# Folding x along the sequence, with the sequence factored as 32 x 94 instead of 64 x 47

## The chip, the cores and the metric

One Trainium2 chip, one of its NeuronCores. The metric is the device time of one launch in microseconds (us). TensorE is PE in the profile, its weight loads PEld; VectorE is DVE, ScalarE ACT, GpSimd POOL, and SyncE SP, which here only issues DMAs.

## The reference

`x` has the shape (2, 3008, 256). The first layer takes the real part of a two-dimensional discrete Fourier transform over the sequence (3008) and the features (256). Its 6016 rows pass a gated layer: rows are scaled to unit mean square (`rms`, with `rms_g`), `silu(xn @ w_gate) * (xn @ w_val) @ w_out` with an inner width of 1536, and then a second layer `h = x @ w_in; (h * cos(h)) @ w_out` with an inner width of 2048. All of it is float32.

```python
X = np.fft.fft(np.fft.fft(x, axis=1), axis=2).real
rms = np.sqrt(np.mean(x * x, axis=-1, keepdims=True) + 1e-06)
silu(xn @ w_gate) * (xn @ w_val) @ w_out      # xn = x / rms * rms_g
g = h * np.cos(h); g @ w_out                  # h = x @ w_in
```

## The kernel before

The transform of a real input is symmetric, so only the rows s and -s are computed as pairs: u is the part that the two share, v the part in which they differ, and the two tokens of a pair are u + v and u - v (`one_token`). The sequence is factored: position n1 * 47 + n2, frequency k1 + 64 * k2, with N1 = 64, N2 = 47; of the k1 only K1 = 33 are needed.

**First stage.** x stands in SBUF as (batch, n1) on 128 partitions. SP loads it in 11 chunks (`load_x`), VectorE folds the features of each chunk in place (L745, L748: x[d] and x[256-d] to their sum and difference), TensorE transforms over n1 (L386; for each of 47 n2 and both halves c of the features a matmul of 132 columns, behind `warm_up` passes), and ScalarE copies the result to `g_sb` (L541). TensorE then waits for `n1_out`, `feat_in` and `seq2_in`.

**Middle.** The loop over G takes two k1 at a time, 17 steps per batch. `features` (L402) transforms over the features (128 and 129 columns for each k1), `pq_copy` (VectorE, L767) takes its result from PSUM and adds the column of feature 128, and `sequence` (L416, L418) of the step before transforms over n2, with 47 and 94 columns. ScalarE copies u and v out (`uv_copy` L550, `row0_copy` L560), squares them for the mean (`square`, L572), and POOL adds the squares of u and v (`add_squares`, L957). `rms` (L430) sums over the features on TensorE, `mean_copy` (L580, L584) moves the means into rows of `stat`, one part at a time: 4 parts per batch, each with an issue of a DMA on ScalarE's queue. `add_epsilon` and `recip` (VectorE), `root` (ScalarE) and `inverse` (POOL) turn them into 1/rms, for three groups of rows.

In the same loop the weights are prepared, at steps that lists fix by hand (`WO1_AT`, `MIX_AT`, `WIN2_AT`). Every float32 weight is split in a rounded high part (ScalarE, L600, L606, L612) and the low rest (POOL, L933). For w1 VectorE first scales the two halves of the rows (L792, L793: `raw_a` by ga and by ga0) and then adds or subtracts the other half (L800, the mix). All 12 parts of w1 and all 6 of wo1 are ready before tile 0; of win2 4 of 8 are, and the others follow in tile 0.

SP's queue is in order: after `inv_done` 1 it stores 1/rms to DRAM (`store_inv`, L289), loads it back spread over the partitions (`load_inv`, L307), stores all of batch 0's u and v (`store_uv`, L298), waits for that (L303), and loads the first tile. POOL scales it (`scale_uv`, L976), ScalarE rounds it (`split_uv`, L616), POOL takes the rest (L1012) and increments `uv_split`, for which TensorE waits before `up1(0, 0)`.

**Tiles.** Six tiles of 502 pairs. In each, `up1` (12 steps of 4 x 3 passes, L442 to L444) computes gate and value, VectorE combines them (L832, L840, L841), ScalarE applies silu (L678), POOL multiplies (L1043), and high and low parts (L639, L817, L933) feed `down` two steps later; then `up2` and `down` do the same for the second layer, over 16 steps, with sin and squares for the cosine. Every product is of three matmuls (high by high, high by low, low by high). One mean, the last, is summed in tile 0, between the first halves of `up1(0, 1)`.

## Time and profile before

| what | value |
|---|---|
| median of 3 runs | 1018.89 us (1018.28 to 1018.94) |
| the profiled execution | 1018.42 us |
| its span, first to last instruction | 1016.7 us |
| busy: TensorE, VectorE, ScalarE, GpSimd | 1008.2, 759.1, 648.2, 368.6 us |
| granted TensorE clock | 1.000 |
| DMA traffic | 32.55 MB |

The times are from the profile; the 1.7 us between span and time lie outside the first and last instruction. A matmul of float32 is shown as two passes (x2). Busy times overlap where an instruction starts before the one in front of it has drained, so the distance of two starts says more than a duration.

### The profile page before, as it was taken

How to read it: one execution, taken by the hardware profiler on the slowest of the kernel's cores; microseconds unless marked ns; L12 is line 12 of the kernel's file. 1: busy time of each engine (PE TensorE's matmuls, PEld its weight loads, DVE VectorE, ACT ScalarE, POOL GpSimd, SP SyncE). 2: the span in 40 equal slices, each digit the busy share in tenths (PEclk: the TensorE clock that was granted, in tenths of full speed). 3: DMA queues.
4: the chain of work that ended last, by engine and by line, in shares of the span. 5: the costliest groups of instructions: out<-in, count | busy, mean ns of one | idle time of the engine just before them, and what ended most of it. 6: DMA issues, size and time to landing. Idle time of an engine off the chain costs nothing.

```text
span 1016.7 us, 13635 instructions
## 1 busy us (share of the span) xinstructions
PE 1008.2 (99%) x4780; PEld 841.4 (83%) x4780; DVE 759.1 (75%) x1059; ACT 648.2 (64%) x850; POOL 368.6 (36%) x302
## 2 busy tenths in 40 slices
PE   8999999999999999999999999999999999999998
PEld 8988788888888888888888888888888888888886
DVE  6785997776887776887676887676887676887665
ACT  6566567876446876446876447876447876447776
POOL 0486887102763002763002763002763002761000
PEclk9999999999999999999999999999999999999999
DMA  9611400000101000101000101000100000100001
GB/s 312 262 42 62 155 1 31 11 1 0 41 1 41 1 1 0 41 0 40 0 0 1 40 0 41 0 0 0 40 1 30 0 0 0 40 0 1 0 0 41
DMA packets 10277, 32.55 MB, mean 32 GB/s; under 512 B 2458, under 2 KB 6298, under 8 KB 9498
## 3 DMA queue, kind: packets, MB, share of 16 engines
q1 hardware_dynamic: 10102, 32.05, 9.0%
q8 instruction: 17, 0.28, 0.1%
q14 instruction: 26, 0.21, 0.1%
q10 hardware_dynamic: 132, 0.01, 0.0%
HBM read 22.78 MB, written 9.26 MB: 32 GB/s over the span
## 4 chain that ended last, share of the span: by engine, by line
PE 97%; DMA 1%; DVE 1%; ACT 0%; issue 0%; POOL 0%; SPq 0%; ACTq 0%; DVEq 0%
PE ps L442 30%; PE ps L443 30%; PE ps L444 30%; PE ps L402 3%; PE ps L418 2%; PE ps L386 2%; PE ps L416 1%; DMA x_sb<-x 1%; PE ps L430 1%; POOL work L1043 0%; SPq L262 0%; DVE pq L767 0%; ACT g_sb L541 0%; DVE dif_f L800 0%; ACT work L678 0%
## 5 line engine op out<-in xcount | busy, mean ns | idle before, releaser
L442 PE MATMUL ps<-h_hi,wo_hi 128*128 128x502 f32 x672 | 261.4, 389 | 0.5 <-DVE h_lo L817 0.5
L444 PE MATMUL ps<-h_hi,wo_lo 128*128 128x502 f32 x672 | 261.6, 389 | 0.0
L443 PE MATMUL ps<-h_lo,wo_hi 128*128 128x502 f32 x672 | 260.9, 388 | 0.0
L933 POOL TENSOR_TENSOR h_lo<-work,h_hi 128x502 fp32r<-128x502 f32 x92 | 101.7, 1114 | 381.0 <-ACT h_hi L654 381.0
L639 ACT ACTIVATE h_hi<-work 128x502 fp32r<-128x502 f32 x132 | 82.7, 626 | 189.3 <-POOL work L1043 189.3
L920 DVE SCALAR_TENSOR_TENSOR work<-work,ps 128x1004 f32<-128x1004 f32 (+1 forms) x109 | 117.2, 1075 | 97.6 <-ACT work L723 97.2
L906 DVE SCALAR_TENSOR_TENSOR work<-work,ps 128x1004 f32<-128x1004 f32 (+1 forms) x109 | 116.5, 1074 | 49.0 <-ACT work L709 49.0
L442 PE MATMUL ps<-x_hi,win_hi 128*128 128x502 f32 x384 | 150.0, 391 | 0.0
L443 PE MATMUL ps<-x_lo,win_hi 128*128 128x502 f32 x384 | 149.4, 389 | 0.0
L444 PE MATMUL ps<-x_hi,win_lo 128*128 128x502 f32 x384 | 149.1, 388 | 0.0
L442 PEld LDWEIGHTS ps<-h_hi,wo_hi 128*128 128x128 f32 x672 | 126.2, 188 | 27.2 <-issue 0.9
L444 PEld LDWEIGHTS ps<-h_hi,wo_lo 128*128 128x128 f32 x672 | 126.3, 188 | 25.8
L443 PEld LDWEIGHTS ps<-h_lo,wo_hi 128*128 128x128 f32 x672 | 126.2, 188 | 25.9
L832 DVE SCALAR_TENSOR_TENSOR plus<-u,w,ps 128x502 f32<-128x502 f32 x144 | 105.8, 734 | 52.1 <-PE ps L444 51.4
L709 ACT ACTIVATE work<-ps 128x1004 f32<-128x1004 f32 (+1 forms) x109 | 98.3, 907 | 60.5 <-PE ps L444 59.6
L718 ACT ACTIVATE work<-work 128x1004 f32<-128x1004 f32 (+1 forms) x109 | 102.7, 943 | 31.6 <-DVE work L906 30.8
L1043 POOL TENSOR_TENSOR work<-work,uv_t 128x502 f32<-128x502 f32 x72 | 99.1, 1397 | 49.5 <-DVE uv_t L841 44.5
L825 DVE TENSOR_TENSOR h_lo<-work,h_hi 128x502 fp32r<-128x502 f32 x172 | 111.1, 684 | 1.4
L654 ACT ACTIVATE h_hi<-work 128x1004 fp32r<-128x1004 f32 (+1 forms) x109 | 101.7, 939 | 14.3 <-PE ps L444 8.7
L723 ACT ACTIVATE work<-work 128x1004 f32<-128x1004 f32 (+1 forms) x109 | 102.8, 943 | 8.0
L1043 POOL TENSOR_TENSOR work<-work,work 128x502 f32<-128x502 f32 x60 | 84.4, 1427 | 36.3 <-DVE work L841 32.5
L442 PEld LDWEIGHTS ps<-x_hi,win_hi 128*128 128x128 f32 x384 | 72.2, 188 | 16.4 <-DVE work L920 1.6
(86 smaller groups left out, 1479.3 us busy)
## 6 DMA issues: line engine op xcount, KB each, us to landing
out<-y_sb SPq DMA_DIRECT2D x10, 502.0 KB, 3.0
x_sb<-x SPq DMA_DIRECT2D x6, 768.0 KB, 10.3
uv_t<-uv_dram SPq DMA_DIRECT2D x6, 502.0 KB, 3.6
uv_dram<-uv SPq DMA_DIRECT2D x2, 1457.0 KB, 8.9
win_raw<-win SPq DMA_DIRECT2D x1, 2048.0 KB, 14.8
wo_raw<-wo SPq DMA_DIRECT2D x1, 2048.0 KB, 9.7
raw_a<-w1a SPq DMA_DIRECT2D x1, 1536.0 KB, 21.9
wo_raw<-wo SPq DMA_DIRECT2D x1, 1536.0 KB, 24.5
```

What stands on the lines that cost most here:

```text
L442: nc.tensor.matmul(acc, w_hi, v_hi, start=start, stop=False)
L443: nc.tensor.matmul(acc, w_hi, v_lo, start=False, stop=False)
L444: return nc.tensor.matmul(acc, w_lo, v_hi, start=False, stop=stop)
L654: nc.scalar.activation(h_hi[j % 2][:, gs, 0:N], work[j % 4][:, gs, :], ACT.Copy).then_inc(hi_done, gs.stop - gs.start)
L718: nc.scalar.activation(work[j % 4][:, gs, :], work[j % 4][:, gs, :], ACT.Sin, scale=TURN / 2).then_inc(sin_done, gs.stop - gs.start)
L723: nc.scalar.activation(work[j % 4][:, gs, :], work[j % 4][:, gs, :], ACT.Square, scale=float(np.sqrt(2.0))).then_inc(sin2_done, gs.stop - ...
L825: nc.vector.tensor_tensor(h_lo[j % 2][:, g, 0:N], work[j % 4][:, g, :], h_hi[j % 2][:, g, 0:N].bitcast(F32), ALU.subtract).then_inc(hid_sp ...
L832: nc.vector.scalar_tensor_tensor(out=plus[m][:, :], in0=u128[:, :], scalar=w128[:, m * C1 + i:m * C1 + i + 1], in1=ps[:, bank_pair(m), 0:N ...
L906: nc.vector.scalar_tensor_tensor(out=buf, in0=buf, scalar=MAGIC, in1=pair, op0=ALU.subtract, op1=ALU.subtract).then_inc(frac_done, gs.stop ...
L920: nc.vector.scalar_tensor_tensor(out=buf, in0=buf, scalar=1.0, in1=pair, op0=ALU.subtract, op1=ALU.mult).then_inc(cos_done, gs.stop - gs.s ...
L933: nc.gpsimd.tensor_tensor(dst, src, hi.bitcast(F32), ALU.subtract).then_inc(s, 1)
L1043: nc.gpsimd.tensor_tensor(work[i % 3][:, g, :], work[i % 3][:, g, :], value[i % 2][:, g, :], ALU.mult).then_inc(h_done[g], 1)
```

## The change

x is folded along the sequence too. The host places x twice, as positions t and -t: on 128 partitions stand (position or its mirror, batch, n1), now with N1 = 32 and, of N2 = 94, the H = 48 first n2; VectorE adds to the features' fold a fold across the two feature orders, and the first transform takes 4 blocks (two folds, two batches) of 34 columns. K1 becomes 17. The tables carry the weight 1/2 where a position is its own mirror.

- First stage: 24 groups m of 512 columns instead of 47 of 256, in 10 chunks; per chunk three operations on VectorE instead of two; 48 matmuls of 136 columns instead of 94 of 132; two warm-up matmuls ahead of every chunk but the first.
- Middle: 34 steps of one k1. `features` keeps 128 and 129 columns, `sequence` has 94 and 188, and runs two steps behind; three PSUM banks for the first, four for the second, four slots of `pq`. ScalarE works on pairs of steps (17), with one split in two where the batches meet.
- Means: 9 parts (3 3 4 4 3 and 4 4 4 5 rows of k1), seven in the loop, two in tile 0.
- w1: `raw_b` is scaled once by gb0 (6 operations), then 12 mixes read `raw_a` and `raw_b` (the 6 others of the scaling are gone). Loads come in the order seq2 (first 8 k1), raw_b, seq2 (rest), wo1, raw_a.
- Half of w1's low parts (6), 2 of wo1's and all of win2 move from the middle into tile 0, on ScalarE and POOL.
- SP stores the first 6 rows of batch 0's u and v early, loads tile 0, stores the rest, and only then stores 1/rms and loads it.

The core of the diff:

```diff
-N1, N2 = 64, 47
+N1, N2 = 32, 94
+H = N2 // 2 + 1
...
-STEPS = (K1 + 1) // 2
-CHUNKS = [1, 2, 3, 3, 6, 6, 6, 6, 6, 6, 2]
+STEPS = K1
+CHUNKS = [1, 2, 3, 3, 3, 3, 3, 3, 2, 1]
+PARTS = [[3, 3, 4, 4, 3], [4, 4, 4, 5]]
...
+        RMS_AT = [8, 10, 14, 18, 22, 26, 30]
+        RMS_LATE = range(len(RMS_AT), MEANS)
...
-        MIX_AT = [6, 7, 9, 10, 12, 13, 15, 16, 18, 19, 21, 22]
-        WO1_AT = [3, 4, 5, 6, 9, 12]
-        WIN2_AT = 24
+        W1_ORDER = [0, 3, 1, 4, 2, 5]
+        SCALE_AT = [5, 6, 7, 8, 9, 10]
+        MIX_AT = [13, 14, 16, 17, 19, 20, 22, 23, 25, 26, 29, 31]
+        W1_HI_AT = [7, 9, 11, 13, 15, 16]
+        WO1_AT = [4, 5, 5, 6]
...
             load(feat[:, :], t_feat, feat_in)
-            load(seq2[0:SEQ_ROWS, :, :], t_seq2.rearrange("p (a k) -> p a k", a=K1), seq2_in)
+            load_seq2(slice(0, SEQ2_FIRST), seq2_in)
+            load(raw_b[:, :], w1b, raw_b_in)
+            load_seq2(slice(SEQ2_FIRST, K1), seq2_rest)
+            load(wo1_raw[:, :], wo1, wo1_in)
             load(raw_a[:, :], w1a, raw_a_in)
-            load(wo1_raw[:, :], wo1, wo1_in)
-            load(raw_b[:, :], w1b, raw_b_in)
...
+            store_uv(0, (slice(0, 1), slice(1, FIRST_ROWS)))
+            sp.wait_ge(uv_stored, UV_FIRST)
+            sp.wait_ge(pq_done, STEPS)
+            load_tile(0)
+            load_u128(0)
+            store_uv(0, (slice(FIRST_ROWS, K1 - 1), slice(K1 - 1, K1)))
             sp.wait_ge(inv_done, 1)
             store_inv(0, (slice(0, 1), slice(1, FIRST_ROWS)), 0)
             sp.wait_ge(inv_out, INV_OUT[0])
             load_inv(0)
-            store_uv(0)
-            sp.wait_ge(uv_stored, 48)
-            sp.wait_ge(pq_done, K1)
-            load_tile(0)
-            load_u128(0)
...
+                if G >= 4:
+                    pe.wait_ge(uv_row0, 2 * (G // 2 - 1))
+                if G == SEQ2_FIRST:
+                    pe.wait_ge(seq2_rest, 16)
+                bank = 4 + G % 4
...
+                if 0 < q < len(RMS_AT):
+                    pe.wait_ge(mean_out, q)
...
+            for G in range(LAST):
                 features(G)
+                if G >= 2:
+                    sequence(G - 2)
+                if G in RMS_AT:
+                    rms(RMS_AT.index(G))
+            sequence(LAST - 2)
...
             pe.wait_ge(uv_split, 1)
-            pe.wait_ge(w1_lo_done, 12)
-            pe.wait_ge(wo1_lo_done, 6)
...
+            for p in range(LAST // 2):
+                uv_copy(p)
+                row0_copy(p)
+                for q in parts_ending(p):
                     square(q)
+                for q in means_copied(p):
                     mean_copy(q)
+                split_step(p)
+                if p == 6:
                     root(0)
+                if p == 13:
                     root(1)
+                if p == 12:
                     split_uv(0)
...
                     if first and i == 0:
+                        for q in RMS_LATE:
+                            mean_copy(q)
+                    if first and i in (2, 3):
+                        wo1_part(WO1_EARLY + i - 2)
+                    if first and 4 <= i < 8:
+                        win2_part(2 * (i - 4))
+                        win2_part(2 * (i - 4) + 1)
...
+                nc.vector.tensor_tensor(part[:, :, 0:DIM], part[:, :, 0:DIM], part[:, :, DIM:XM], ALU.add
+                                        ).then_inc(even_done, 1)
+                dve.wait_ge(even_done, i + 1)
...
+            for G in range(LAST):
                 pq_copy(G)
                 split_step(G)
+                if G == 14:
                     add_epsilon(0)
+                if G == 16:
                     recip(0)
+                if G == 27:
                     add_epsilon(1)
+                if G == 30:
                     recip(1)
...
+                    if first and i < 6:
+                        w1_part(W1_EARLY + i)
+                    if first and 6 <= i < 8:
+                        wo1_part(WO1_EARLY + i - 6)
+                    if first and 8 <= i < 10:
+                        win2_part(i - 8)
```

`means_copied(p)` gives mean q to the pair p = (RMS_AT[q] - 2) / 2, and `parts_ending(p)` gives each part's square to the pair that holds its last row. On POOL the middle's order is now: `add_squares` 0, 1, wo1 0, squares 2, wo1 1 and 2, squares 3, wo1 3, `inverse(0)`, w1 0 and 1, squares 4, w1 2 and 3, squares 5, `scale_uv(0)`, `scale_u128(0)`, the low part of uv, squares 6, w1 4 and 5, squares 7, `inverse(1)`, squares 8. Behind `x2_ready` in tile 0 it has the 8 parts of wo2 and 6 of win2.

## Rows read from the trace of the kernel before

**Rows 1.** Page: busy time of the engines (share of the span).

```profile
PE 1008.2 (99%) x4780; PEld 841.4 (83%) x4780; DVE 759.1 (75%) x1059; ACT 648.2 (64%) x850; POOL 368.6 (36%) x302
```

**Rows 2.** Windows by stage: length, busy us (count) by engine, granted clock, DMA share, GB/s.

```profile
0.00:29.90 29.90, 26.67 (x204) 25.92 (x204) 16.25 (x28) 19.76 (x34) 0.20 (x4) 1.00 0.94 316
...
29.90:94.70 64.80, 64.32 (x539) 58.52 (x539) 49.05 (x94) 38.14 (x108) 48.10 (x42) 1.00 0.31 120
...
165.00:1016.70 851.70, 847.79 (x3737) 701.02 (x3735) 632.22 (x845) 551.08 (x655) 270.18 (x217) 1.00 0.04 12
```

**Rows 3.** Timeline of the first stage: TensorE, then VectorE (start, length, instruction).

```profile
12.02 17.34 PE L386 MATMUL ps<-seq,x_sb 128*128 128x132 f32 x152 [1.58 <-DVE x_sb L748]
...
29.91 2.00 PE L402 MATMUL ps<-feat,g_sb 128*94 128x129 f32 x16 [0.55 <-ACT g_sb L541]
...
20.39 0.95 DVE L745 TENSOR_TENSOR x_sb<-x_sb 128x762 f32<-128x762 f32 x1 [0.96 <-DMA x_sb<-x]
...
22.25 0.42 DVE L745 TENSOR_TENSOR x_sb<-x_sb 128x254 f32<-128x254 f32 x1
```

**Rows 4.** DMA issues up to 60 us, SP's timeline, and a window (columns as above).

```profile
seq<-t_seq SPq DMA_DIRECT2D x1, 1163.2 KB, 18.9
...
9.12 0.45 SPq L262 DMA_DIRECT2D seq<-t_seq  x1
...
20.00:27.00 7.00, 7.00 (x65) 7.00 (x64) 3.10 (x8) 6.08 (x11) 0.00 (x0) 1.00 0.96 220
```

**Rows 5.** Timeline of TensorE in the middle: one step and one mean.

```profile
32.61 1.05 PE L402 MATMUL ps<-feat,g_sb 128*94 128x129 f32 x8
...
33.49 0.32 PE L416 MATMUL ps<-seq,pq 94*128 94x47 f32 x2
...
33.91 0.35 PE L416 MATMUL ps<-seq,pq 94*128 94x47 f32 x2
...
45.31 0.79 PE L430 MATMUL ps<-squares,consts 128*1 128x376 f32 x2
```

**Rows 6.** ScalarE by line and shape in the middle (busy, mean ns, idle before), and its timeline.

```profile
L550 ACT ACTIVATE uv<-ps 128x188 f32<-128x188 f32 x32 | 10.5, 327 | 23.9 <-PE ps L418 23.9
...
L572 ACT ACTIVATE squares<-uv 128x752 f32<-128x752 f32 x6 | 5.0, 832 | 0.2
...
L606 ACT ACTIVATE wo_hi<-wo_raw 128x512 fp32r<-128x512 f32 x6 | 3.7, 623 | 0.0
...
57.29 0.63 ACTq L584 DMA_DIRECT2D stat<-mean_row  x1
```

**Rows 7.** VectorE in the middle, by line and shape, and its timeline.

```profile
L767 DVE SCALAR_TENSOR_TENSOR pq<-feat,ps 94x256 f32<-94x256 f32 x66 | 29.5, 476 | 20.5 <-PE ps L402 20.5
...
L800 DVE SCALAR_TENSOR_TENSOR sum_f<-raw_b,gvec,sum_f 128x512 f32<-128x512 f32 x6 | 6.3, 1054 | 0.0
...
66.06 0.44 DVE L782 RECIPROCAL stat<-stat 16x47 f32<-16x47 f32 x1 [0.47 <-ACT stat L590]
...
70.28 1.76 DVE L800 SCALAR_TENSOR_TENSOR sum_f<-raw_b,gvec,sum_f 128x512 f32<-128x512 f32 x1
```

**Rows 8.** SP's waits (total, times, longest), a DMA issue, POOL's timeline.

```profile
SPq L307 <- DMA inv_dram<-stat: 1.0, 1, 1.0
...
SPq L303 <- DMA uv_dram<-uv: 5.7, 1, 5.7
...
inv_t<-inv_dram SPq DMA_DIRECT2D x6, 251.0 KB, 3.2
...
83.53 2.28 POOL L976 TENSOR_TENSOR uv_t<-uv_t,inv_t 128x502 f32<-128x502 f32 x2 [0.67 <-DMA uv_t<-uv_dram]
```

**Rows 9.** Timeline of tile 0: POOL, then TensorE.

```profile
112.63 1.08 POOL L933 TENSOR_TENSOR h_lo<-work,h_hi 128x502 fp32r<-128x502 f32 x1
...
114.91 2.96 POOL L1043 TENSOR_TENSOR work<-work,work 128x502 f32<-128x502 f32 x2
...
105.89 0.46 PE L442 MATMUL ps<-h_hi,wo_hi 128*128 128x502 f32 x1 [0.53 <-DVE h_lo L817]
```

More of the change, by code:

```diff
@@ L28 @@
 assert ITEMS % 2 == 0 and C2 % 4 == 0
-STEPS = (K1 + 1) // 2
-CHUNKS = [1, 2, 3, 3, 6, 6, 6, 6, 6, 6, 2]
-SEQ_ROWS = 96
-assert sum(CHUNKS) == N2 and 2 * N2 <= SEQ_ROWS <= P
+STEPS = K1
+FOLD = 2 * BATCH * N1
+CHUNKS = [1, 2, 3, 3, 3, 3, 3, 3, 2, 1]
+assert FOLD == P and sum(CHUNKS) * 2 == H and 2 * H <= P
 FEAT = 2 * P + 1
-MEANS = STEPS // 4
+PARTS = [[3, 3, 4, 4, 3], [4, 4, 4, 5]]
+assert all(sum(p) == K1 for p in PARTS)
+MEANS = sum(len(p) for p in PARTS)
 MAGIC = 1.5 * 2.0 ** 23
@@ L43, in tables @@
     one = np.stack([np.cos(a), -np.sin(a)], axis=2).reshape(N1, 2 * K1)
-    seq1 = np.zeros((BATCH, N1, BATCH, 2 * K1))
-    for b in range(BATCH):
+    seq1 = np.zeros((2 * BATCH, N1, 2 * BATCH, 2 * K1))
+    for b in range(2 * BATCH):
         seq1[b, :, b] = one
@@ L204, in mean_cols @@
-        def mean_cols(i):
-            return slice(8 * i * N2, (8 * (i + 1) if i < MEANS - 1 else K1) * N2)
-        PART_END = [b * STEPS + (4 * i + 3 if i < MEANS - 1 else STEPS - 1)
-                    for b in range(BATCH) for i in range(MEANS)]
-        def parts_ending(G):
-            return [q for q, end in enumerate(PART_END) if end == G]
+        COLS1 = 2 * BATCH * 2 * K1
+        LAST = BATCH * STEPS
+        PART_ROWS = [(b, slice(sum(PARTS[b][:i]), sum(PARTS[b][:i + 1])))
+                     for b in range(BATCH) for i in range(len(PARTS[b]))]
@@ L228, in stat_rows @@
+        assert PART_ROWS[1][1].stop == FIRST_ROWS and sum(TAKE[:FIRST_ROWS]) >= N
         def stat_rows(b, k):
@@ L376, in _ @@
             pe.wait_ge(seq1_in, 16)
-            for g, n2s in enumerate(GROUPS):
+            for g, ms in enumerate(GROUPS):
                 for c in range(2):
@@ L505, in tile @@
                 up1(t, 1, halves=(1,))
+                if first:
+                    rms(RMS_LATE[1])
                 if not first:
@@ L1047, in tile @@
                     lo1(t, i, 1, hid_ready_first)
-                    if first and i in (2, 4, 6, 8):
-                        win2_part(WIN2_EARLY + i // 2 - 1)
+                    if first and i < 6:
[4 more added lines that the diff above has]
+                        win2_part(i - 8)
                 pool.wait_ge(x2_ready, 4 * (t + 1))
                 if first:
-                    for k in range(8):
+                    wo2_part(0)
+                    win2_part(2)
+                    win2_part(3)
+                    wo2_part(1)
+                    wo2_part(2)
+                    win2_part(4)
+                    win2_part(5)
+                    wo2_part(3)
+                    wo2_part(4)
+                    win2_part(6)
+                    win2_part(7)
+                    for k in (5, 6, 7):
                         wo2_part(k)
@@ L1097 @@
                             up[P].reshape(2 * C1, P).T], axis=1)
+    t = np.arange(N1)[:, None] * N2 + np.arange(H)[None, :]
+    ahead = x[:, t][..., np.concatenate([first, second])]
+    behind = x[:, -t % SEQ][..., np.concatenate([[0], second[1:], [P], first[1:]])]
+    both = np.stack([ahead, behind], axis=3).reshape(BATCH, N1, H // 2, 2, 2 * DIM)
     arrays = {
-        "x": np.ascontiguousarray(x[:, :, np.concatenate([first, second])].reshape(BATCH * N1, N2 * DIM)),
+        "x": np.ascontiguousarray(both.transpose(3, 0, 1, 2, 4).reshape(P, H // 2 * 2 * DIM)),
         "w1a": np.ascontiguousarray(up[first]), "w1b": np.ascontiguousarray(up[second]),
```

416 lines of the change are left out of this document (204 added, 212 removed).

## Prediction

> **What bounds the kernel now.** I read the page first: TensorE is busy for 99% of the span [rows 1]; its granted clock is 1.00 in every stretch, the 2.4 GHz level [rows 2]. So only less TensorE work, or less waiting in front of it, shortens the run. The windows by stage then say where that can be [rows 2]. Of 1016.7 us, 851.7 lie behind 165 us and are not touched; the 70.3 ahead of it are tile 0's first half; the change works on the 29.9 us of the first stage and the 64.8 us of the middle (features, sequence, means). In the middle TensorE is busy for 64.3 us, VectorE for 49.1, ScalarE for 38.1 and POOL for 48.1: three helpers with slack, which a TensorE cut in half would use up. A run of 1018.42 us was profiled; the median is 0.47 above it, and I forecast against the median.
>
> **First stage: 4.0 us less.** Its TensorE work falls from 94 matmuls of 132 columns (two passes each, 152 passes in 17.34 us, 0.114 a pass [rows 3]) to 48 of 136: 48 x 2 x 0.114 x 136/132 = 11.3 us, from 21.4. But then TensorE no longer ends the stage; two other things do.
> (a) The folding on VectorE. A 762-column operation takes 0.95 us, a 254-column one 0.42 [rows 3], so about 1.04 ns a column and 0.16 fixed. A chunk of 3 now needs 768 + 381 + 381 columns, 2.07 us, for the same 768 KB for which two operations took 1.9. Six such chunks from 8.5 to 9 us (3 MB of x have then landed halfway between today's chunks) end at 21.5; the chunk of 2 adds 1.6, that of 1 adds 1.05: 24.2. Four matmuls (0.94) and the last copy (today TensorE is idle for 0.55 us at the same place [rows 3]) give 25.8.
> (b) The wait for seq2 before the first feature pass. Today seq2 is issued at 9.12 and lands 18.9 later, at 28.0; while feat and seq2 move, the queues carry 220 GB/s [rows 4], against 316 over the whole stage [rows 2]. The first part is now 0.58 MB of 1.19: 0.61/0.220 = 2.8 us earlier, less 0.3 to 0.4 for 0.13 MB more x: 25.6.
> They nearly tie; I take 25.9 for today's 29.91. Bounds: 24.4 if the chunks land earlier than VectorE needs, 28.0 if the split of seq2 brings nothing.
>
> **The middle on TensorE alone.** Today one k1 costs 0.44 us of features (8 passes for two k1 in 0.88, from 32.61 to 33.49) and 0.43 of sequence: 47- and 94-column passes both take about 0.11 us, since four passes go by in 0.42 to 0.45 us whatever their width [rows 5]. That is 128 columns' worth; a weight load takes its place when the data is narrower. So the 94-column pair stays at 0.22, while 188 columns scale from the 129-column passes (0.11 x 188/129 = 0.16) to 0.32. With 34 k1 instead of 66: features 15.0, sequence 33 x 0.54 = 17.8 before the first tile. Seven means lie in the loop; one of 376 columns costs 0.8 [rows 5], one of 282 some 0.65 by its columns: 5.2. Sum 38.0 us, against 64.8 today. Halved passes aren't a halved time, because the widest one becomes wider than its weight load.
>
> **What the helpers make of it.** ScalarE per pair of k1: copy of 376 columns 0.55 (0.327 for 188 [rows 6], 0.2 more for twice), row 0 in 0.3: 0.85, 17 times: 14.5, with 0.5 for the split pair. Nine squares of 0.6 to 0.9 (0.83 at 752) 6.8; seven mean copies at some 0.5 and 0.63 for the DMA issue [rows 6], 1.15 each: 8.1; 12 + 4 weight copies of 0.62, some 0.1 of it beside the next, 8.4; the roots and the split of uv 1.5. That is 39.4 us of work in a stage of 38.0: ScalarE is a second bound, where it waited 23.9 us today [rows 6]. VectorE: 34 pq copies at 0.45 (0.476 less what overlaps) 15.3, six scalings at about 0.55 3.3, twelve mixes at 1.05 12.6 [rows 7], epsilon and reciprocals 2.7: 34 us, where it waited 20.5 us today. Its mixes aren't of one length: their mean is 1.05, and one beside a POOL operation took 1.76 [rows 7]. The waits between them, in us after the first feature pass:
> - mean 1 waits for mean copy 0, which stands behind a pair's copies: 0.45 lost.
> - recip(0) stands at step 16 on VectorE and waits for root(0), last in ScalarE's pair 6. ScalarE is in arrears from pair 4 (3.3 us of work) and 6 (3.6): root(0) ends at 21.4, VectorE gets there at 19.2. It is blocked for 2.2 with pq_copy(17) queued behind, and TensorE loses 1.3 (today the same wait is 0.47 [rows 7]).
> - root(1) stands in pair 13, behind split_uv in pair 12. ScalarE reaches split_uv at 36.0. Its data: recip(0) 21.9, inverse on POOL 24.4; SP then first issues the rest of batch 0's uv (ready at 24.8), now ahead of store_inv (26.5). Today store_inv, two issues of 0.35, is waited for 1.0 us with nothing ahead, and the store of uv is waited for 5.7 us after its last issue [rows 8]. Taken as landing behind it, inv is out at 30.7, loaded 3.2 later and scaled in 2.28 [rows 8]: 36.3. I take this end, since the two are issued back to back. So split_uv ends at 37.5, root(1) at 39.7, and recip(1), at step 30 of VectorE, holds back pq_copy(31) and (32) until 42.1; sequence(32) ends at 42.7, where up1(0, 0) starts. uv_split itself is there at 39.8.
> So the middle takes 42.7 us, 22.1 less. Bounds: 38.5 if nothing waits, 47.5 if each mix takes the 1.76 us that one of them took [rows 7] (12 x 0.7 = 8.5, half of it on the path).
> The row shows store_inv, alone, landing within 1.0 us of its issue. The Trainium skill ("DMA: Bandwidth & Descriptors", Queues, rings and completion order) says that a semaphore increment lands only after every earlier write of its DMA engine; it speaks against the new order on SP. By that rule the middle is 42.7; by the row with nothing ahead inv comes 4 us sooner, ScalarE alone sets the pace and it is 42.2. No row of before has the two stores in this order.
>
> **Tile 0: 1.0 us more.** A second late mean adds 0.85 on TensorE. ScalarE has two mean copies between silu(0) and h_hi(0) (1.15 more, of which some was idle); TensorE already waits 0.53 at down(0) [rows 9]. Both overlap: +0.6. POOL gets six w1, two wo1 and two win2 parts in i = 0 to 9, where there were four win2 parts. Its load per i is 2.5 to 2.96 for the products and 2.28 for h_lo and a weight part (112.63 to 114.91) [rows 9], 4.8 to 5.2 us against TensorE's 5.4 (24 passes x 0.227), and i = 1 has only 2.7 to 4.2; its products come 1 to 2 us late for a few i, against 1 to 2 us of slack in front of h_lo on VectorE: +0.4. The parts after x2_ready (14 x 1.38 = 19.3 us, from 11.0) are each due later than they end, and scale_uv(1) then ends 6 us ahead of its split: nothing. If that cover goes, a late part costs TensorE its own 1.4 us. Bounds: 0 and +4 (ten parts at 0.4 late each).
>
> **Sum:** -4.0 - 22.1 + 1.0 = -25.1; 1018.89 - 25.1 = 993.8 us.
>
> **Rivals.**
> 1. Helpers block each other more (chance 0.22, 999 us). The price is 5 us: the inverse chain late by as much, which split_uv passes on to copies, root(1) and VectorE, or VectorE's mixes at 1.5 us. For: three engines within 4 us of one another, all in order, and two or four buffers between them. Against: POOL's share of the stage hardly rises, from 48 of 65 us to some 34 of 43.
> 2. Less waiting than I walked through (0.12, 989.5 us): the middle at 39.5 and the first stage at 25. For: the sum of TensorE alone; against: ScalarE's 39.4.
> 3. Slower than before: TensorE at its lower level (0.03, 1032 us). Place: the first stage, where it is now fed only about 15 of 24 us with warm-up passes, and the gap before the features. Price: at 1.2 GHz all 38.0 us of the middle would be 76 + 5, so +16 there, with -4 and +1: +13. From about two thirds of the middle at half pace on, 25 us, the gain is gone. Against: the granted clock is 1.00 in every window [rows 2], and behind the 1.58 us idle that end at 12.02 the passes still came at 0.114 [rows 3].
> 4. The change is made but wide passes cost more than their width (in rival 1): 0.2 us on each of 34 would be 7 us.
>
> **How the numbers follow.** Forecast 0.62 (own range 990 to 997), rivals 0.22, 0.12, 0.03, and 0.01 for no change. About 0.2%, 2 us, is what a measurement can tell from none. Adding the bounds gives 987 and 1003; both ends at once are unlikely, and the likelier errors are waits, so I give 988.5 to 1001. Faster 0.96, same 0.01, slower 0.03.
>
> **What would show it.** The first feature pass at 25 to 27 us, after a wait on seq2 or a copy of about 1 us; 0.97 us per k1 where nothing waits; up1(0, 0) at 67 to 70; VectorE idle for ScalarE's stat twice, over 2 us each, and ScalarE nearly without idle; down(0) waiting for h_lo by about 1 us; nothing changed behind tile 0. I am wrong if the middle is over 47 us, if up1 waits for uv_split, or if POOL holds TensorE in tile 0 for over 4 us.

## The result, and the profile after

The changed kernel takes 1008.13 us in the median of four runs (1007.69 to 1010.11), the kernel before 1018.91 beside it: a ratio of 0.990, 95% interval 0.9881 to 0.9919. One of the four runs of the kernel before took 1046.06 us, and the ratio leaves it out. The change saves 10.8 us where 25.1 were forecast, and the time lies outside the forecast range of 988.5 to 1001. The profiled execution took 1008.31 us, with a span of 1006.5. First the page of the changed kernel, busy time by engine:

```profile
PE 985.5 (98%) x4464; PEld 815.2 (81%) x4464; DVE 752.1 (75%) x1028; ACT 636.7 (63%) x804; POOL 366.1 (36%) x303
```

TensorE is busy for 22.7 us less than before [rows 1]. But the span shrank by 10.2 only, so there is now idle time. The windows by stage (columns as in [rows 2]) find it: first stage, middle, the part behind 165 us, and then a stretch of the middle:

```profile
0.00:26.15 26.15, 21.81 (x142) 20.21 (x142) 17.32 (x35) 9.77 (x18) 0.20 (x4) 1.00 0.93 325
26.15:82.50 56.35, 44.73 (x282) 38.11 (x283) 35.11 (x56) 28.14 (x62) 26.96 (x27) 0.88 0.45 156
165.00:1006.50 841.50, 838.41 (x3694) 692.95 (x3692) 628.34 (x835) 542.35 (x639) 269.67 (x216) 1.00 0.04 13
46.00:50.00 4.00, 4.00 (x22) 3.95 (x21) 1.74 (x4) 2.00 (x4) 1.70 (x3) 0.58 0.13 15
```

The first stage ends at 26.15. The middle takes 56.35 us, not 42.7: TensorE is idle for 11.62 of them, and its granted clock is 0.88 in the mean, 0.58 in the stretch shown and 0.50 from 62 to 66 us, near and at the 1.2 GHz level, where it was 1.00 before. Out of the list of waits of the whole run (us in total, times, longest), TensorE's two of the middle, and ScalarE's for the sequence passes:

```profile
PE ps L462 <- issue: 9.1, 3, 4.3
PE ps L448 <- DVE pq L822: 2.1, 1, 2.1
...
ACT uv L587 <- PE ps L450: 25.0, 12, 5.3
```

L462 is `rms`, the matmul that sums the squares for a mean; L448 and L450 are `sequence`, whose result ScalarE's `uv_copy` (L587) takes. And the timeline of TensorE, from the first feature pass to `up1(0, 0)` at 82.50 and the first wait of tile 0:

```profile
26.15 1.56 PE L433 MATMUL ps<-feat,g_sb 128*96 128x129 f32 x12 [0.60 <-ACT g_sb L576]
28.14 0.60 PE L433 MATMUL ps<-feat,g_sb 128*96 128x129 f32 x4
29.13 0.60 PE L433 MATMUL ps<-feat,g_sb 128*96 128x129 f32 x4
...
37.36 0.63 PE L462 MATMUL ps<-squares,consts 128*1 128x282 f32 x2 [0.44 <-ACT mean_row L625]
...
44.92 0.79 PE L462 MATMUL ps<-squares,consts 128*1 128x376 f32 x2 [2.81 <-issue]
...
46.39 0.57 PE L448 MATMUL ps<-seq,pq 96*128 96x94 f32 x2
...
49.79 0.36 PE L448 MATMUL ps<-seq,pq 96*128 96x94 f32 x2
...
58.37 0.63 PE L462 MATMUL ps<-squares,consts 128*1 128x282 f32 x2 [2.02 <-issue]
...
61.72 0.74 PE L448 MATMUL ps<-seq,pq 96*128 96x94 f32 x2 [2.10 <-DVE pq L822]
...
76.82 1.41 PE L462 MATMUL ps<-squares,consts 128*1 128x376 f32 x2 [4.25 <-issue]
...
82.50 0.52 PE L474 MATMUL ps<-uv_hi,sum_hi 128*128 128x502 f32 x1
...
95.23 0.47 PE L474 MATMUL ps<-h_hi,wo_hi 128*128 128x502 f32 x1 [1.76 <-DVE h_lo L873]
```

One k1 costs 0.99 us where nothing waits (28.14 to 29.13). The five bracketed waits of the middle, 0.44, 2.81, 2.02, 2.10 and 4.25, are its 11.62 us idle. Behind the four long ones passes take much longer: 0.57 for the first sequence pass at 46.39, 0.36 for the same one at 49.79 (and 0.89 against 0.51 for the wider one). They aren't always the first passes: the mean and the features right behind the 2.02 still came at full pace (0.63 and 0.68), and the granted clock fell only 1.2 us behind that wait, as the next one began.

"issue" as the releaser of `rms` names no engine, so the producer has to be found by the times: a matmul of `rms` waits for `sq_added`, which POOL increments. So POOL's timeline around the three waits, and behind it ScalarE's squares for the first of the three:

```profile
42.75 1.27 POOL L989 TENSOR_TENSOR wo_lo<-wo_raw,wo_hi 128x512 fp32r<-128x512 f32 x1 [7.05 <-ACT wo_hi L645]
43.97 0.85 POOL L1015 TENSOR_TENSOR squares<-squares 128x376 f32<-128x376 f32 x1
...
55.15 1.25 POOL L989 TENSOR_TENSOR sum_lo<-sum_f,sum_hi 128x512 fp32r<-128x512 f32 x1
56.37 1.25 POOL L989 TENSOR_TENSOR dif_lo<-dif_f,dif_hi 128x512 fp32r<-128x512 f32 x1
57.60 0.68 POOL L1015 TENSOR_TENSOR squares<-squares 128x282 f32<-128x282 f32 x1
...
73.64 2.28 POOL L1060 TENSOR_TENSOR uv_lo<-uv_t,uv_hi 128x502 fp32r<-128x502 f32 x2 [3.38 <-ACT uv_hi L663]
75.87 0.85 POOL L1015 TENSOR_TENSOR squares<-squares 128x376 f32<-128x376 f32 x1
```

```profile
40.18 0.83 ACT L617 ACTIVATE squares<-uv 128x752 f32<-128x752 f32 x1
```

ScalarE's squares are done at 41.0, and for the two others at 54.9 and 71.5. POOL adds them at 43.97, 57.60 and 75.87 and `rms` starts as each addition ends. In between POOL stood, in its own order, at a part of wo1 whose high half ScalarE had not rounded (7.05 idle), at w1 parts, and at `uv_lo`, waiting 3.38 for ScalarE's `uv_hi`. In the kernel before, POOL's first sum was ready at 41.37, 3.9 us ahead of the mean at 45.31 [rows 5]:

```profile
40.22 1.15 POOL L957 TENSOR_TENSOR squares<-squares 128x376 f32<-128x376 f32 x1
```

Last, VectorE's timeline of the changed kernel:

```profile
45.69 0.42 DVE L830 TENSOR_SCALAR stat<-stat 6x94 f32<-6x94 f32 x1 [2.87 <-DMA stat<-mean_row]
...
54.95 6.32 DVE L856 SCALAR_TENSOR_TENSOR dif_f<-raw_a,gvec,raw_b 128x512 f32<-128x512 f32 x1
61.98 0.74 DVE L856 SCALAR_TENSOR_TENSOR sum_f<-raw_a,sm,raw_b 128x512 f32<-128x512 f32 x1
...
75.72 0.73 DVE L836 RECIPROCAL stat<-stat 11x94 f32<-11x94 f32 x1 [3.10 <-ACT stat L634]
```

One mix takes 6.32 us, from 54.95 to 61.27; the next of the same size 0.74. POOL worked with no gap of 0.1 us or more from 51.30 to 60.71, and the mix ended 0.56 us after that. Two mixes that fell beside the small first operations of that run, at 52.39 and 53.84, took only 0.73 and 0.78. The copy of `pq` queued behind it is what TensorE waits 2.10 us for at 61.72.

### The profile page after: what moved, and what is told of

Its sections match the earlier page's. It is cut to its first block, busy times and chain, and to the rows that moved or that the text cites. A ratio compares the mean times of both kernels' runs of the same rounds, so it can differ in the third digit from the quotient of the medians.

```text
span 1006.5 us, 12914 instructions
## 1 busy us (share of the span) xinstructions
PE 985.5 (98%) x4464; PEld 815.2 (81%) x4464; DVE 752.1 (75%) x1028; ACT 636.7 (63%) x804; POOL 366.1 (36%) x303
## 4 chain that ended last, share of the span: by engine, by line
PE 93%; issue 2%; ACT 1%; POOL 1%; DVE 1%; DMA 0%; ACTq 0%; SPq 0%; DVEq 0%; POOLq 0%
PE ps L474 30%; PE ps L476 29%; PE ps L475 29%; PE ps L418 1%; PE ps L433 1%; PE ps L450 1%; POOL work L1091 1%; PE ps L448 1%; DMA x_sb<-x 0%; PE ps L462 0%; PE ps L404 0%; ACT uv L587 0%; DVE pq L822 0%; POOL dif_lo L989 0%; POOL sum_lo L989 0%
## 5 line engine op out<-in xcount | busy, mean ns | idle before, releaser
L476 PEld LDWEIGHTS ps<-h_hi,wo_lo 128*128 128x128 f32 x672 | 126.2, 188 | 25.9
L881 DVE TENSOR_TENSOR h_lo<-work,h_hi 128x502 fp32r<-128x502 f32 x172 | 114.1, 702 | 1.5
L1091 POOL TENSOR_TENSOR work<-work,uv_t 128x502 f32<-128x502 f32 x72 | 99.2, 1399 | 43.2 <-DVE uv_t L897 40.1
```

The source lines that it names most:

```text
L476: return nc.tensor.matmul(acc, w_lo, v_hi, start=False, stop=stop)
L881: nc.vector.tensor_tensor(h_lo[j % 2][:, g, 0:N], work[j % 4][:, g, :], h_hi[j % 2][:, g, 0:N].bitcast(F32), ALU.subtract).then_inc(hid_sp ...
L1091: nc.gpsimd.tensor_tensor(work[i % 3][:, g, :], work[i % 3][:, g, :], value[i % 2][:, g, :], ALU.mult).then_inc(h_done[g], 1)
```

## The experiments

The theories: **A**, the means wait because the sums of squares stand late in POOL's in-order queue; **B**, the helpers' load as such bounds the middle, so a wait removed comes back elsewhere; **C**, the idle stretches drop the clock and the passes behind them cost extra; **E**, a VectorE operation with two SBUF inputs is held as long as POOL works without a pause. "Up1" below is the start of `up1(0, 0)`, 82.50 in the changed kernel. What follows it is nearly the same in every run: span less up1 is 924.0 in the changed kernel and 923.3 to 924.1 in all kernels below, so up1 tells nearly all. The kernel before took 1018.8 to 1019.6 us in the same sessions; intervals are those of the ratio to it.

**1. Squares first.** `add_squares` 2, 4 and 6 each go ahead of the weight part or `uv_lo` in front of them.

```diff
+            add_squares(2)
             wo1_part(0)
-            add_squares(2)
...
+            add_squares(4)
             w1_part(0)
             w1_part(1)
-            add_squares(4)
...
             scale_u128(0)
+            add_squares(6)
             pool.wait_ge(uv_hi_done, 1)
...
-            add_squares(6)
             w1_part(4)
```

> Edit: on POOL the sums of squares 2, 4 and 6 are put ahead of wo1 part 0, of w1 parts 0 and 1, and of the low part of uv. Theory A (the means wait on POOL's order: in the changed kernel TensorE idled 2.81, 2.02 and 4.25 us in front of means 2, 4 and 6, and its passes ran at half pace for 2 to 3 us behind each): these three idle stretches go, and with them most of the half-paced passes; the VectorE instruction of 6.3 us beside POOL may stay. Middle 43 to 47 us instead of 56.4, time 996 to 1000 us. Rival B (ScalarE and VectorE are saturated, the mean is only where it shows): the waits move to pq and uv copies, middle over 52 us, time over 1004 us.

Measured: 1001.54 us, 0.9817 (0.9794 to 0.9839); up1 at 76.06. Two of TensorE's waits in the middle, and VectorE's longest mix:

```profile
42.49 0.79 PE L462 MATMUL ps<-squares,consts 128*1 128x376 f32 x2 [0.46 <-issue]
...
58.52 0.74 PE L448 MATMUL ps<-seq,pq 96*128 96x94 f32 x2 [4.18 <-DVE pq L822]
```

```profile
51.75 6.31 DVE L856 SCALAR_TENSOR_TENSOR dif_f<-raw_a,gvec,raw_b 128x512 f32<-128x512 f32 x1
```

A holds: two of the three mean waits fall to 0.46, and the third is gone. The time is 1.5 us above what A expected and 2.5 below what B did: the mix is still held, and TensorE, which comes to it earlier, waits 4.18 for `pq` instead of 2.10.

**2. Only squares 2 first.**

> Edit: only the sum of squares 2 is put ahead of wo1 part 0 on POOL. Theory A: the 2.81 us in front of mean 2 go, but VectorE stands in add_epsilon(0) until the mean's DMA has landed (4.3 us after its issue), so that pq_copy(15) is still late by about 1 us: 2 to 4 us less than the changed kernel, half-paced passes behind it included, 1004 to 1006 us. Rival B: under 1 us less.

Measured: 1004.92 us, 0.9845 (0.982 to 0.987); up1 at 79.73. The time is as A expected. But in the profiled execution no mix took over 1.51 us, so part of the 3.2 us is not this edit's; and TensorE now waits 2.21 us, where about 1 was expected, for a copy of `pq` that stands behind `add_epsilon(0)`, which waited 2.75 for the mean's DMA.

**3. TensorE kept at work.** Spare matmuls into the bank of the means, 12, 9 and 19 of them, stand ahead of the waits of means 2, 4 and 6.

```diff
-                pe.wait_ge(sq_added, q + 1)
                 if 0 < q < len(RMS_AT):
                     pe.wait_ge(mean_out, q)
+                for _ in range({2: 12, 4: 9, 6: 19}.get(q, 0)):
+                    nc.tensor.matmul(ps[:, 3, 0:P], feat[:, 0:P], feat[:, 0:P], start=True, stop=True)
+                pe.wait_ge(sq_added, q + 1)
```

> Edit: TensorE runs 12, 9 and 19 spare 128-column matmuls into the mean's bank in front of its waits for the sums of squares 2, 4 and 6, so that it doesn't idle there; POOL's order is untouched. Theory C (the clock: each idle stretch is followed by passes at the lower level, 1.2 GHz): the passes behind the three waits come at full pace, the idle stretches stay as they are in length but filled; 3 to 4 us less than the changed kernel, 1004 to 1005 us (what follows the wait for pq, 2.1 us idle, stays slow). Rival D (the slow passes come from contention in the memories, not from the clock): they stay slow, time the same or up to 1 us more.

Measured: 1007.67 us, 0.9873 (0.9849 to 0.9897); up1 at 82.07. TensorE's passes right behind the filled wait at mean 2:

```profile
45.73 0.79 PE L464 MATMUL ps<-squares,consts 128*1 128x376 f32 x2 [0.95 <-POOL squares L1017]
...
46.97 0.36 PE L448 MATMUL ps<-seq,pq 96*128 96x94 f32 x2
```

The passes are at full pace, 0.36 where it was 0.57, and the releaser is now named: POOL's squares. So C is right on the cause of the slow passes (memory contention, the expectation's rival D, would have left them slow), and wrong on the price, 0.5 us instead of 3 to 4: TensorE only came earlier to the next wait (mean 5 waited 1.66 for its squares, and sequence 2.14 for `pq`). Half pace costs time only where nothing else is late.

**4. A pause for POOL.** POOL waits for the sixth mix before w1's part 2, in the changed kernel (`e5_gap`), and before part 0 in the kernel of experiment 1 (`e6_gap`).

```diff
+            pool.wait_ge(mixed, 6)
             w1_part(2)
```

> Edit: POOL waits for VectorE's sixth mix before w1 part 2, so that its run of seven operations without a pause (52.5 to 60.7 us) has a gap. Theory E (a VectorE operation with two inputs in SBUF gets no access while POOL runs without a pause: the mix of 6.3 us ended when POOL's run did): the mix ends with POOL's operation before the gap, 3 to 4 us sooner, TensorE's wait for pq of 2.1 us goes: 3 to 4 us less than the changed kernel, 1004 to 1005 us. Rival F (POOL and VectorE share the access evenly, and the length of the mix has another cause): the mix stays over 5 us and the time is the same within 1 us.

> Edit: on top of the squares put first, POOL waits for VectorE's sixth mix before w1 part 0, which ends its run (49.3 to 57.5 us there) in front of the four w1 parts. Theory E (a VectorE operation with two inputs in SBUF is held while POOL runs without a pause): the mix that took 6.31 us there takes under 2 us, TensorE's 4.18 us wait for pq goes, and with it the half-paced passes behind it (59 to 64 us, some 2.5 us lost): 5 to 7 us less than with the squares alone, 995 to 996.5 us. Rival F (the length of that mix has another cause): 1001 to 1002 us, unchanged.

Measured: 1007.43 us, 0.9875 (0.985 to 0.9901), up1 at 82.58; and 1002.15 us, 0.9836 (0.9802 to 0.9869), up1 at 75.95. The longest mix of the first, and then of the second:

```profile
56.56 3.87 DVE L856 SCALAR_TENSOR_TENSOR dif_f<-raw_a,gvec,raw_b 128x512 f32<-128x512 f32 x1
```

```profile
53.51 6.59 DVE L856 SCALAR_TENSOR_TENSOR sum_f<-raw_a,sm,raw_b 128x512 f32<-128x512 f32 x1
```

In the first the mix ends after 3.87 us, 0.55 behind POOL's last operation before the wait, and TensorE's wait of 2.10 for `pq` is gone. That is E. No time is gained all the same: the wait at mean 2, which stands ahead of the edit, was 3.46 in this execution instead of 2.81, and the mean clock of the middle was 0.85 instead of 0.88. In the second the edit did not do what it was meant to: mix 6, at 51.76, took 0.88 and was done before POOL came to the wait, so POOL never paused, and the next mix was held until 60.10, again 0.55 behind POOL's run, which ended at 59.55. It says nothing on what a pause does.

**5. Two late pieces.** On top of `e6_gap`: ScalarE's last high parts of w1 behind `silu(1)` in tile 0 (`e7_silu_early`), and with that `recip(1)` at step 32 instead of 30 (`e8_recip_late`).

> Edit: on top of the gap, the rounding of the last two w1 parts (1.04 us of ScalarE in front of the first silu) goes behind silu(1) of tile 0. Theory G (TensorE's 1.5 us wait for h_lo at down(0), 0.53 before, is set by the chain from ScalarE's last pair through silu(0)): about 0.9 us less than with the gap, wait at down(0) 0.5 to 0.8 us. Rival H (the chain through the two late means or POOL's last sum of squares sets it): no change, within 0.2 us.

> Edit: on top of silu early, VectorE takes recip(1) at step 32 instead of 30, so that pq_copy 31 and 32 don't stand behind root(1). Theory (the second of the waits in the prediction, root(1) on ScalarE holding VectorE for 3.1 us, costs TensorE what is seen of it: 0.6 + 0.3 us in front of sequence 31 and 32): about 0.9 us less than with silu early. Rival: ScalarE's copies of u and v end just as late, and nothing is gained, within 0.3 us.

Measured: 1001.45 us, 0.9813 (0.9784 to 0.9843), and 1000.83 us, 0.982 (0.9787 to 0.9852). The first takes the wait at `down(0)` from 1.52 to 0.94 us: 0.6 of the 2.0 us that tile 0 takes more is ScalarE's order there. Of the second the runs lay from 997.96 to 1003.48 us, too far apart to show the 0.9 us expected, though the 0.61 us in front of the last sequences is gone from its trace. Its profiled execution, one of the short ones, held no mix at all, though POOL had the same work:

```profile
53.47 1.29 POOL L991 TENSOR_TENSOR sum_lo<-sum_f,sum_hi 128x512 fp32r<-128x512 f32 x1 [0.63 <-DVE dif_f L858]
...
56.44 2.00 POOL L991 TENSOR_TENSOR sum_lo<-sum_f,sum_hi 128x512 fp32r<-128x512 f32 x1
```

```profile
55.63 1.39 DVE L858 SCALAR_TENSOR_TENSOR dif_f<-raw_a,gvec,raw_b 128x512 f32<-128x512 f32 x1
```

Here the two engines take turns: POOL's part takes 2.00 instead of 1.25, VectorE's mix 1.39. And here the wait for mix 6 did stop POOL, for 0.63 us up to 53.47. So the amount of POOL's work alone doesn't decide whether a mix is held; experiment 8 sets two runs of one kernel side by side.

**6. seq2 in one piece**, on `e7_silu_early`.

> Edit: on silu early, with seq2 loaded in one piece ahead of raw_b, as before the change. Theory (the prediction's (b): the wait for seq2 decides when it is 2.8 us later than with the split): the first feature pass comes at 28 to 28.5 us instead of 26.1, 2 to 2.3 us more than silu early. Rival (the folding alone sets the start, the split of seq2 brings nothing): start unchanged, same time.

Measured: 999.94 us, 0.9807 (0.9777 to 0.9837). The first feature pass:

```profile
27.70 1.53 PE L432 MATMUL ps<-feat,g_sb 128*96 128x129 f32 x12 [1.98 <-DMA seq<-t_seq]
```

It starts at 27.70 where the other kernels start at 25.7 to 26.6, so the split brings about 1.4 us at the start. The whole is not 2 us longer, as the theory had it: up1 came at 74.71, against 76.72, with no held mix (again POOL had paused for mix 6, up to 54.84). How the middle goes weighs more than where it starts.

**7. Later means, and another order of POOL.** `e12_lag_only` is the changed kernel with each mean two steps later and nothing else. `e10_pool_order` is `e1` with the pieces of 5, squares 5 earlier and waits on single mixes between the w1 parts; `e11_pool_and_lag` is both.

```diff
-        RMS_AT = [8, 10, 14, 18, 22, 26, 30]
+        RMS_AT = [8, 12, 16, 20, 24, 28, 32]
```

> Edit: the changed kernel, means two steps of k1 later and nothing else; POOL's order stays as the change has it. Theory (the mean waits for the squares in POOL's in-order queue, 9.1 us in three waits): each of the three waits falls by about 2 us, and with them some of the passes at half pace, so up1(0, 0) at 75 to 79 instead of 82.5 and the whole at 999 to 1004 us. Rival (the helpers' load bounds the middle, the means only show it): the waits turn up elsewhere, 1007 to 1008 us.

> Edit: the squares before each late weight part on POOL as in e1_squares_first, w1_hi(5) behind silu(1), recip(1) at step 32, and POOL's orders between squares 4 and 6 written so that the w1 parts no longer stand in one run: each of w1 0 to 3 waits until VectorE's mix 7, 8, 9, 10 is done, squares 5 stand ahead of w1 2, squares 6 ahead of uv_lo. Theory (the middle lost its time to means waiting for POOL's squares, to one VectorE mix held for 6.3 us through a pause-free run of POOL, and to passes at half pace behind the idle stretches): no mix over 2 us, no mean that waits over 1 us, no pass at half pace; up1(0, 0) at 70 to 71 instead of 76.1 in e1, and the whole at about 995 us. Rival (the helpers' work as such is what bounds the middle, so whoever is freed makes another late): POOL, waiting for the mixes, comes late with scale_uv(0) and uv_lo, up1(0, 0) stays at 74 or later and the whole at 999 us or more.

> Edit: e10_pool_order with the means two steps of k1 later (steps 12, 16, 20, 24, 28, 32 where the change has 10, 14, 18, 22, 26, 30), so that each has two steps of about 1 us more for its sum of squares. Theory: what is left of waiting at the means in e10 (some 0.4 to 1 us in sum) goes, so 0 to 2 us less than e10. Rival: the later means only put VectorE's epsilon and reciprocals later, which then hold pq copies: as much as e10 or up to 2 us more.

Measured: 999.43 us, 0.9827 (0.9788 to 0.9867); 998.73 us, 0.9793 (0.9767 to 0.9819); 999.9 us, 0.9807 (0.979 to 0.9823). A single list of steps gives 8.7 of the missing 14 us, the lower end of what was expected; `e10_pool_order` is 3.7 above its theory and just below its rival, and `e11_pool_and_lag` gains nothing on it. In the profiled executions up1 is at 70.18, 72.96 and 76.27. In the last, TensorE waits 3.13 us for ScalarE's copies, which stand behind `split_uv`, which waits 3.56 for POOL's scaling: what the rival of `e10_pool_order` (POOL comes late through the waits on mixes) foresaw. The runs of `e12_lag_only` lay from 995.91 to 1005.95 us, and the shortest was the profiled one.

**8. The same kernel again**, to see what a long run does.

> No edit: the same kernel as e12_lag_only, whose runs lay between 995.9 and 1006.0 us, profiled and timed once more, to see what differs between a short and a long run of one kernel. Theory: a long run holds one VectorE mix for over 3 us beside POOL and has passes at half pace behind the idle stretches it makes (clock below 1.00 in the middle), a short one has neither; behind up1(0, 0) the two take the same time within 0.5 us. Rival: the difference lies elsewhere (loads that land later, or behind tile 0), with the middle alike within 1 us.

Measured: 1000.45 us, 0.9816 (0.9802 to 0.9829); the profiled run took 1003.6, up1 at 77.98. The stretch of the held mix, first in the profiled run of `e12_lag_only` (995.91 us), VectorE and then POOL:

```profile
53.50 2.36 DVE L856 SCALAR_TENSOR_TENSOR sum_f<-raw_a,sm,raw_b 128x512 f32<-128x512 f32 x1
```

```profile
56.94 1.72 POOL L989 TENSOR_TENSOR dif_lo<-dif_f,dif_hi 128x512 fp32r<-128x512 f32 x1
```

and in that of `e14_lag_again`, VectorE, POOL, and what TensorE made of it (timeline, and the window 58 to 62):

```profile
52.76 10.04 DVE L856 SCALAR_TENSOR_TENSOR sum_f<-raw_a,sm,raw_b 128x512 f32<-128x512 f32 x1
```

```profile
56.77 1.25 POOL L989 TENSOR_TENSOR dif_lo<-dif_f,dif_hi 128x512 fp32r<-128x512 f32 x1
...
61.02 1.23 POOL L1039 TENSOR_TENSOR u<-u,inv_t 128x502 f32<-128x502 f32 x1
```

```profile
63.25 0.74 PE L448 MATMUL ps<-seq,pq 96*128 96x94 f32 x2 [6.33 <-DVE pq L822]
```

```profile
58.00:62.00 4.00, 0.00 (x0) 0.00 (x0) 4.00 (x1) 0.00 (x0) 4.00 (x5) 0.57 0.00 0
```

One mix takes 10.04 us and ends at 62.80, 0.55 after POOL's run, 9.8 us of it from the first w1 part at 52.45 on, ends at 62.25. POOL works at 1.25 to 1.26 an operation, as if VectorE weren't there; TensorE and ScalarE do nothing for four us. In the short run the same mix takes 2.36, POOL pays with up to 1.72 a part, and the clock stays at 1.00. Behind up1 both took 923.8 to 923.9, so the 7.7 us between these two runs lie in the middle (up1 at 77.98 against 70.18), where the held mix and the half pace behind it are. The longer runs of the other kernels left no trace, so that they have the same cause isn't shown.

**9. All together.** `e12_lag_only`, squares 6 first, the pieces of 5, and the first rows' epsilon, root and reciprocal two steps later (`e13_together`); then POOL's order rewritten, with waits that were meant to keep its runs short (`e15_mix_gaps`, the part of its diff that concerns POOL):

```diff
             inverse(0)
+            add_squares(4)
+            pool.wait_ge(mixed, 7)
             w1_part(0)
+            pool.wait_ge(mixed, 8)
             w1_part(1)
-            add_squares(4)
-            w1_part(2)
-            w1_part(3)
             add_squares(5)
             scale_uv(0)
+            pool.wait_ge(mixed, 9)
             scale_u128(0)
+            pool.wait_ge(mixed, 10)
+            w1_part(2)
+            add_squares(6)
             pool.wait_ge(uv_hi_done, 1)
...
-            add_squares(6)
+            w1_part(3)
             w1_part(4)
```

> Edit: e12_lag_only, and with it squares 6 ahead of uv_lo on POOL, w1_hi(5) behind silu(1), recip(1) at step 32, and the chain of the first rows' statistics two steps later on all its engines (epsilon at step 16, root in pair 7, reciprocal at step 18), so that the mean's DMA, which took over 4 us beside the bulk loads, has landed when VectorE comes to it. Theory (the middle is bounded by TensorE alone once the in-order queues are free of these waits): the 1.47 us at step 15, the 1.94 us at mean 6 and 0.6 of the 1.56 us at down(0) go, up1(0, 0) at 66 to 68 instead of 70.2, the profiled time at 991 to 993 us where VectorE is not held, and the median at 993 to 998. Rival (what is taken away there comes back as waits of VectorE and POOL on each other, as it did in e6_gap): up1(0, 0) at 70 or later, the median at 999 us or more.

> Edit: e13_together, with POOL's order between the inverse and uv_lo rewritten: squares 4 first, then w1 0 after mix 7, w1 1 after mix 8, squares 5, scale_uv(0), after mix 9 scale_u128(0), after mix 10 w1 2, squares 6; w1 3 behind uv_lo. So POOL never has more than about 5 us of work without a wait on VectorE, and neither squares 4 nor scale_uv(0) stands behind a weight part. Theory (in e12, e13 and e14 the time above the forecast is VectorE's mix, or POOL's small operations, held by the other of the two through a run without a wait: 10.0 us in e14, 4.5 in e13): no VectorE mix over 3 us, no wait of TensorE over 2 us in the middle, granted clock 1.00 there, up1(0, 0) at 66 to 69, and the median at 992 to 996 us with the runs within 3 us of one another. Rival (the two engines hold each other in any order, and the waits on the mixes only make POOL late): a mix or a POOL operation of over 3 us again, the median at 998 to 1000.

Measured: 999.13 us, 0.9815 (0.9799 to 0.9831), and 996.46 us, 0.9772 (0.9734 to 0.9811), with six runs within 2.5 us. `e13_together` came out as its rival had it (up1 at 73.75): the DMA wait is gone, but in the profiled execution mean 4 waited 4.01 us for squares that stood behind the inverse and two weight parts, and a mix was held for 4.50. `e15_mix_gaps`, waits of TensorE in the middle, longest mix, and the whole middle as one window:

```profile
55.80 0.64 PE L462 MATMUL ps<-squares,consts 128*1 128x282 f32 x2 [1.57 <-issue]
67.31 0.79 PE L462 MATMUL ps<-squares,consts 128*1 128x376 f32 x2 [1.69 <-issue]
70.82 0.46 PE L474 MATMUL ps<-uv_hi,sum_hi 128*128 128x502 f32 x1 [1.02 <-POOL dif_lo L991]
```

```profile
57.49 2.03 DVE L858 SCALAR_TENSOR_TENSOR sum_f<-raw_a,sm,raw_b 128x512 f32<-128x512 f32 x1
```

```profile
26.08:70.82 44.74, 39.95 (x283) 33.58 (x283) 30.49 (x56) 28.78 (x64) 29.94 (x25) 1.00 0.53 191
```

No mix over 2.03 us, no wait over 1.69, the clock at 1.00: as expected, though up1 at 70.82 is later and the median 0.5 us above what was expected. It is the best of these kernels, 22.5 us less than before. POOL is what TensorE waits for in all three rows (its sums for the two means ended at 55.70 and 67.21). But the four new waits are not shown to be the reason: each mix was done before POOL came to the wait for it. POOL still worked from 50.05 to 58.97 with hardly a gap, and what then stopped it, for 0.78 us, was the DMA of 1/rms. What did change is the order of its pieces and so what fell beside the mixes.

## Why the prediction was wrong

**The first stage was right.** The first feature pass starts at 26.15, forecast 25.9, bounds 24.4 to 28.0; the releaser is the last copy of `g_sb`, path (a), and seq2 in one piece would have made it 27.70.

**TensorE's own work was nearly right.** One k1 costs 0.99, forecast 0.97. Where the clock stayed up the middle's busy time was 40.1 us in `e12_lag_only` and 39.95 in the window above, against 38.0; the slower features behind each of the seven means (0.68 instead of 0.60) account for some of the 2 us; the rest wasn't taken apart.

**The step that failed is "What the helpers make of it".** It listed three waits of VectorE and ScalarE and gave the middle 4.7 us for them. The profile shows 11.62 us idle, and 4.6 more (44.73 busy, less the 40.1) that go with passes at half pace: 40.1 + 11.6 + 4.6 = 56.3. This is how the time passed, and not what each piece would give back: in experiment 3 most passes were at full pace and 0.5 us was gained. In detail:
- The prediction walked through ScalarE's and VectorE's queues and never through POOL's. It wrote "POOL's share of the stage hardly rises" as an argument against rival 1, a statement on load; the loss is from order. Before, `rms` stood five steps of two k1, 5 x 1.74 = 8.7 us, behind the features of the last rows it sums. Now mean 2 sums rows up to k1 = 9 and stands at step 14, five steps of one k1, 4.9 us. The lists still leave five or six steps; the time in them fell nearly to half, about as much as POOL's sum had to spare before (3.9 us), with the same squares (0.83 and 0.85) and weight parts (0.63 and 1.25) to fit in. The prediction took over the steps and never checked the lag. It cost 9.1 us of waiting in three places; moving the squares took 6.6 us off the time, moving the means 8.7.
- ScalarE was counted as a second bound, with 39.4 us of work, "nearly without idle". Its work in the middle, the issues of DMAs included, was 33.1 us here and 33.3 in `e12_lag_only`, and it waited for TensorE's sequence passes for 24.3 us here and 10.1 there. The copies of u and v took 12.0 us instead of 15.0, and 12 of the 16 weight copies, 7.2 us, fell ahead of tile 0. What mattered of ScalarE was the place of single pieces in its order, such as `uv_hi`, for which POOL waited 3.38 us.
- The held mix. The row with 1.76 beside a POOL operation was seen [rows 7], and used as the ceiling for a mix. Where one was held it took 3.9 to 10.0 us. TensorE idled 2.10 us for it here, 4.18 and 6.33 in other runs.
- Half pace. This was rival 3's mechanism at a chance of 0.03, looked for in the first stage, where it didn't come: the stage's clock is 1.00. It came behind the idle stretches that the other errors made. The row it was argued from, 1.58 us idle and full pace behind it [rows 3], agrees with the runs: longer idle stretches than that had not been in the trace.

**Single waits.** Mean 1's 0.45 was there (0.44). `recip(0)` waited 1.74 and `recip(1)` 3.10, forecast at over 2 each, but they did not set the pace. Not foreseen was epsilon(0), 2.87 us for the mean's DMA: issued at 41.32, while the queues moved 428 GB/s (38 to 42 us), it let VectorE go on at 45.69. The new schedule has this small DMA beside the bulk loads; before, it was issued at 57.29 [rows 6], when the queues were all but idle. That the loads are what made it slow is argued from this and not tested. Where mean 2 no longer waited, TensorE lost up to 2.52 us to it (2.21 in `e2_square2_first`, 2.22 in `e10_pool_order`, 2.52 in `e11_pool_and_lag`, 1.47 in `e12_lag_only`), and in `e13_together`, with epsilon two steps later, nothing. The inverse chain, of which the prediction made a main path, bound nothing: SP issued the load of 1/rms at 59.24, it took 3.1, and scaling started at 65.88 behind `add_squares(5)`, which waited for ScalarE. SP's two stores of 1/rms went out from 55.22 on, behind the store of uv at 54.28, and were in by 59.24: 1.9 us after their last issue, where alone it took 1.0 [rows 8]. That fits the order rule weighed there, but it changed nothing in the sum.

**Tile 0** took 2.0 us more (924.0 against 922.0 from up1 to the end of the span), forecast 1.0. The second late mean is 0.9 of it, as costed; the wait at `down(0)` grew from 0.53 [rows 9] to 1.76 instead of 1.13, and moving one piece of ScalarE's work gave 0.6 back. POOL's ten added parts cost nothing that shows.

**Of the rivals**, 1 named the right kind (helpers block each other, 999 us), and one of its two members, long mixes; the other, the inverse chain, bound nothing, POOL's order isn't in it, and its 5 us are a third of the 14 that were missing. The lowest of the changed kernel's runs, 1007.69 us, is above both its time and the range. With the means two steps later the change comes close to the forecast in its shortest run, 995.91 us with up1 at 70.18 where 67 to 70 was forecast; the medians of that kernel, 999.43 and 1000.45, are within the range and about 6 us above the forecast.

**What stays open.** Experiments 4 and 8 show that a mix is held and for how long; why POOL and VectorE take turns in one run and one is held in the next isn't settled: no run varied their order of issue alone. In the three profiles in which a wait for the mix really stopped POOL for 0.63 us (`e5_gap` at 59.89, `e8_recip_late` at 52.84, `e9_seq2_whole` at 54.21) the two took turns behind it, mixes of 1.18 to 1.39 beside POOL's parts of 1.71 to 2.00; and in `e10_pool_order`, where such waits stopped POOL twice, no mix took over 1.02. That points at the pause as the remedy, but four profiles don't prove it. The Trainium skill ("SBUF — State Buffer", Who interferes with whom) says that VectorE's second SBUF input comes through a read port that it shares with GpSimd, that this shared pair is an exclusive lock, and that the order of issue decides who blocks. The rows agree in that the two-input mixes are held while the copies of `pq`, with one of their inputs in PSUM, take 0.38 to 0.48 us throughout. They show more than the page says: a mix waits not for one instruction of 1.25 us but for POOL's whole chain of them, up to 9.8 us.

## What to carry to other kernels

When a stage is cut in half, walk through every in-order queue that feeds it, not only through the busy times: for each sum or split ask what stands ahead of it in its engine's order and what that waits for, and put the piece that TensorE waits for first. A lag written in steps is a lag in time: where the steps get shorter, it has to grow. Look twice at long runs of GpSimd without a pause beside VectorE operations that read two SBUF tiles; where you put in a wait to break one, check in the trace that it stopped the engine at all. Judge such a kernel by several runs, since one trace may show either of its courses.
